# A relative-position bias made by four engines: double evacuations, a moved table load and other shares of the last tiles

## The reference

```python
batch, n_heads, seq, head_dim = 4, 8, 576, 64      # hidden = 32
scores = scale * np.matmul(q, k.transpose(0, 1, 3, 2))
rel = (pos[:, None] - pos[None, :]).astype(np.float32)
x = (np.log1p(np.abs(rel)) / psi_i)[..., None]
h = np.maximum(x @ w1 + b1, 0.0)                   # (seq, seq, 32)
bias = h @ w2                                      # (seq, seq, n_heads)
scores = scores + bias.transpose(2, 0, 1)[None]
attn = softmax(scores);  out = np.matmul(attn, v)
...
# then, on 2304 rows of 512: out += P[:, e:e+1] * (np.maximum(x @ w1[e], 0) @ w2[e]), e < 8
```

## Time and profile before

| what | value |
|---|---|
| median of 3 runs | 1846.01 us (1845.95 to 1847.39) |
| profiled execution | 1847.22 us, its span 1845.4 us |
| busy: PE, DVE, ACT, POOL | 99%, 57%, 45%, 56% of the span |
| granted TensorE clock, mean | 0.999 |
| bias part | from 5.4 us to the first scores at 61.3 us |

### The profile page before, as it was taken

How to read it: one execution, slowest core, us unless ns; L and a number is a source line. 1 busy time by engine, 2 the same in 40 slices (tenths; PEclk the granted TensorE clock), 3 DMA queues, 4 the chain that set the end, 5 groups by cost and what they waited for, 6 DMA issues and landing times.

```text
span 1845.4 us, 27892 instructions
## 1 busy us (share of the span) xinstructions
PE 1829.7 (99%) x10223; PEld 1592.1 (86%) x10223; DVE 1053.4 (57%) x1784; ACT 824.8 (45%) x1416; POOL 1028.3 (56%) x720
## 2 busy tenths in 40 slices
PE   8999999999999999999999999999999999999999
PEld 4677777788999999999999999999999999999998
DVE  8877777777554555456645554555455445544553
ACT  8777777533433333334333333333333333333331
POOL 0223326577666666666776666666666666666661
PEclk9999999999999999999999999999999999999999
DMA  7763562021112211212121211111121111112110
GB/s 241 226 155 92 128 152 68 23 79 59 69 69 69 69 69 69 69 69 103 69 69 69 69 69 69 69 69 69 69 103 69 69 69 69 69 69 69 69 46 35
DMA packets 44127, 152.47 MB, mean 83 GB/s; under 512 B 9584, under 2 KB 18032, under 8 KB 29680
## 3 DMA queue, kind: packets, MB, share of 16 engines
q1 hardware_dynamic: 44016, 150.99, 25.5%
HBM read 135.63 MB, written 15.34 MB: 82 GB/s over the span
## 4 chain that ended last, share of the span: by engine, by line
PE 94%; DVE 1%; ACT 1%; issue 0%; POOL 0%; ACTq 0%; DVEq 0%; POOLq 0%
PE banks L660 14%; PE banks L661 14%; PE banks L659 14%; PE banks L627 13%; PE banks L631 13%; PE banks L629 13%; PE banks L557 4%; PE banks L518 3%; PE banks L500 3%; PE banks L501 2%; PE banks L571 1%; PE banks L528 0%; DVE h_lo L1167 0%; PE banks L678 0%; ACT probs L786 0%
## 5 line engine op out<-in xcount | busy, mean ns | idle before, releaser
L1279 POOL TENSOR_TENSOR w_lo<-stage,w_hi 128x1024 fp32r<-128x1024 f32 (+1 forms) x288 | 647.5, 2263 | 526.8 <-ACT w_hi L832 525.9
L1161 DVE TENSOR_TENSOR u<-p_copy,banks 128x384 f32<-128x384 f32 x192 | 106.4, 554 | 633.3 <-PE banks L631 633.3
L661 PE MATMUL banks<-w_hi,h_lo 128*128 128x512 f32 x1152 | 450.1, 391 | 0.0
L660 PE MATMUL banks<-w_lo,h_hi 128*128 128x512 f32 x1152 | 449.9, 391 | 0.0
L659 PE MATMUL banks<-w_hi,h_hi 128*128 128x512 f32 x1152 | 449.0, 390 | 0.0
L1167 DVE SCALAR_TENSOR_TENSOR h_lo<-corner,h_hi 128x384 fp32r<-128x384 f32 x384 | 411.1, 1098 | 0.0
L879 ACT ACTIVATE h_hi<-corner 128x384 fp32r<-128x384 f32 x384 | 196.5, 526 | 271.1 <-DVE corner L1161 268.1
L627 PE MATMUL banks<-x_hi,w_hi 128*128 128x384 f32 x896 | 300.6, 336 | 0.6 <-DVE u L1161 0.6
L631 PE MATMUL banks<-x_hi,w_lo 128*128 128x384 f32 x896 | 300.2, 335 | 0.0
L832 ACT ACTIVATE w_hi<-stage 128x1024 fp32r<-128x1024 f32 (+1 forms) x288 | 271.6, 974 | 9.1 <-POOL stage L1273 9.1
L868 ACT ACTIVATE p_copy<-banks 128x384 f32<-128x384 f32 x96 | 47.3, 492 | 491.2 <-PE banks L631 491.2
(11 more groups left out here) (130 smaller groups left out, 2478.3 us busy)
## 6 DMA issues: line engine op xcount, KB each, us to landing
stage<-in_expert_w SPq DMA_DIRECT2D x96, 1024.0 KB, 4.7
raw<-in_qk SPq DMA_DIRECT2D x32, 576.0 KB, 7.1
bias_scratch<-bias_out SPq DMA_DIRECT2D x36, 288.0 KB, 2.6
bias<-bias_scratch SPq DMA_DIRECT2D x16, 288.0 KB, 2.9
v_main<-in_v SPq DMA_DIRECT2D x16, 256.0 KB, 2.7
bias<-bias_scratch SPq DMA_DIRECT2D x16, 256.0 KB, 4.0
out<-total SPq DMA_DIRECT2D x4, 768.0 KB, 4.0
out<-total SPq DMA_DIRECT2D x6, 256.0 KB, 2.0
```

The lines of the kernel that those rows point to most:

```text
L660: pe.matmul(dst, h_hi[:, g % 2, f, tokens], lo[:, f], start=False, stop=False)
L661: mm = pe.matmul(dst, h_lo[:, g % 2, f, tokens], hi[:, f], start=False, stop=fp == FPAIRS - 1 and f == 1)
L1161: dve.tensor_tensor(out, other, bank, op).then_inc(combined, 1)
L1279: pool.tensor_tensor(lo, of, hi.bitcast(F32), ALU.subtract).then_inc(w_split, 1)
```

## The change

ScalarE first does a dummy Relu on a column of `ones`, ahead of its waits, so that the activation table is loaded then. It runs two tiles ahead, and evacuates two tiles in one instruction of 128 x 1152 out of four banks, waiting for both tiles' matmuls and both slots' stores. In the last four tiles VectorE makes two units a tile and ScalarE two; these tiles have their own shift column `shift_last`. `bias_tile` on TensorE gets other waits for them, and the last round is written out after the loop. The low part of the first queries is made in two pieces: 128 columns of each head before the keys' low part, the rest after it, signalled by `first_split`, for which TensorE waits before step 1 and SyncE before `pairs_of`. Batch 1 is rounded by ScalarE, ahead of the exps of steps 0 and 1, in place of VectorE. VectorE no longer waits for `attn_consts_in` there.

```diff
+LAST_ROUND = BIAS_TILES - ROUND
+ON_VECTOR_LAST = GROUPS - 2
 # SyncE
+            sp.wait_ge(first_split, 1)
             with sp.Fori(0, PAIRS - 1) as hp:
                 pairs_of(hp, False)
 # TensorE
-            def bias_tile(m, slot):
+            def bias_tile(m, slot, last=False):
                 for first in range(0, GROUPS, 2):
-                    if first + 1 < ON_VECTOR:
+                    if last and first == 0:
+                        pe.wait_ge(hid_vec, ON_VECTOR * LAST_ROUND + ON_VECTOR_LAST * (slot + 1))
+                    elif last:
+                        pe.wait_ge(hid_act, LAST_ROUND + (GROUPS - ON_VECTOR_LAST) * (slot + 1))
+                    elif first + 1 < ON_VECTOR:
+            for slot in range(ROUND):
+                pe.wait_ge(bias_evac, LAST_ROUND - ROUND + slot + 1)
+                bias_tile(LAST_ROUND + slot, slot, last=True)
+                if not exists(hp, s - 2) and exists(hp, s - 1):
+                    pe.wait_ge(first_split, 1)
 # ScalarE
+            act.wait_ge(ones_set, 1)
+            act.activation(col_sum[:, 0:1], ones[:, 0:1], ACT.Relu).then_inc(warm, 1)
             act.wait_ge(consts_in, 48)
-            def keep_bias(m, slot, again=True):
-                act.wait_ge(bias_mm, GROUPS * (m + 1))
+            def keep_bias(m, slot, again=True, offset=shift):
+                act.wait_ge(bias_mm, GROUPS * (m + 2))
                 if again:
-                    act.wait_ge(bias_stored[slot], 16 // ROUND * (m - slot))
-                act.activation(halves(bias_out[:, slot, :]), banks[:, 2 * slot:2 * slot + 2, 0:HALF], ACT.Identity,
-                               bias=shift[:], scale=1.0 / SCALE).then_inc(bias_evac, 1)
+                    for of in range(2):
+                        act.wait_ge(bias_stored[slot + of], 16 // ROUND * (m - slot))
+                act.activation(bias_out[:, slot:slot + 2, :].rearrange("p t (a s) -> p (t a) s", a=2),
+                               banks[:, 2 * slot:2 * slot + 4, 0:HALF], ACT.Identity,
+                               bias=offset[:], scale=1.0 / SCALE).then_inc(bias_evac, 2)
-            for m in range(AHEAD):
+            for m in range(2):
                 hidden_units(m, m, again=False)
+            for m in range(LAST_ROUND - ROUND, BIAS_TILES, 2):
+                for of in range(2, 4):
+                    if m + of < BIAS_TILES:
+                        hidden_units(m + of, (m + of) % ROUND,
+                                     on_vector=ON_VECTOR_LAST if m + of >= LAST_ROUND else ON_VECTOR)
+                keep_bias(m, m % ROUND, offset=shift_last if m >= LAST_ROUND else shift)
             for s in range(STEPS):
+                if s < 2:
+                    round_pair(1, 1, s)
                 step(0, s)
 # VectorE
+            for slot in range(ROUND):
+                hidden_units(LAST_ROUND + slot, slot, again=True, on_vector=ON_VECTOR_LAST)
-            dve.wait_ge(attn_consts_in, 16)
             dve.wait_ge(rounded, 2)
+            split_first_queries(slice(0, P), split_done)
             dve.tensor_tensor(k_lo[0][:, :, :], raw[:, 0, 1, :, :], qk_hi[0][:, 1, :, :].bitcast(F32),
                               ALU.subtract).then_inc(split_done, 1)
+            split_first_queries(slice(P, S), first_split)
             for s in range(STEPS):
                 step(0, s)
-                if s < 2:
-                    dve.wait_ge(raw_in[1], 32)
-                    dve.tensor_copy(qk_hi[1][:, :, s, :], raw[:, 1, :, s, :]).then_inc(rounded, 1)
```

More of the change, by code:

```diff
@@ L473, in _ @@
                 bias_tile(m, m)
-            with pe.Fori(1, BIAS_TILES // ROUND) as i:
+            with pe.Fori(1, BIAS_TILES // ROUND - 1) as i:
                 for slot in range(ROUND):
@@ L736, in _, with hidden_units @@
         def _(act):
+            act.wait_ge(ones_set, 1)
+            act.activation(col_sum[:, 0:1], ones[:, 0:1], ACT.Relu).then_inc(warm, 1)
             act.wait_ge(consts_in, 48)
             act.wait_ge(bias_prep, 3)
-            def hidden_units(m, slot, again=True):
-                j = ON_VECTOR
+            def hidden_units(m, slot, again=True, on_vector=ON_VECTOR):
                 if again:
                     act.wait_ge(bias_mm, GROUPS * (m - ROUND + 1))
-                start = LTAB - S - GROUPS * GROUPS * m - GROUPS * j
-                act.activation(hidden[:, GROUPS * slot + j, :], table[:, bass.ds(start, S)], ACT.Relu,
-                               bias=b1_col, scale=slopes[:, bass.ds(GROUPS * m + j, 1)]).then_inc(hid_act, 1)
-            def keep_bias(m, slot, again=True):
-                act.wait_ge(bias_mm, GROUPS * (m + 1))
-                if again:
-                    act.wait_ge(bias_stored[slot], 16 // ROUND * (m - slot))
-                act.activation(halves(bias_out[:, slot, :]), banks[:, 2 * slot:2 * slot + 2, 0:HALF], ACT.Identity,
-                               bias=shift[:], scale=1.0 / SCALE).then_inc(bias_evac, 1)
+                for j in range(on_vector, GROUPS):
+                    start = LTAB - S - GROUPS * GROUPS * m - GROUPS * j
+                    act.activation(hidden[:, GROUPS * slot + j, :], table[:, bass.ds(start, S)], ACT.Relu,
+                                   bias=b1_col, scale=slopes[:, bass.ds(GROUPS * m + j, 1)]).then_inc(hid_act, 1)
+            def keep_bias(m, slot, again=True, offset=shift):
+                act.wait_ge(bias_mm, GROUPS * (m + 2))
+                if again:
+                    for of in range(2):
[3 more added lines that the diff above has]
+                               bias=offset[:], scale=1.0 / SCALE).then_inc(bias_evac, 2)
             def round_pair(n, slot, h):
@@ L760, in round_pair @@
                 act.activation(qk_hi[slot][:, :, h, :], raw[:, slot, :, h, :], ACT.Copy).then_inc(rounded, 1)
-            for m in range(AHEAD):
+            for m in range(2):
                 hidden_units(m, m, again=False)
-            act.wait_ge(shift_kept, 2)
-            for m in range(ROUND):
-                hidden_units(m + AHEAD, (m + AHEAD) % ROUND, again=m + AHEAD >= ROUND)
+            act.wait_ge(shift_kept, 4)
+            for m in range(0, ROUND, 2):
+                for of in range(2, 4):
+                    hidden_units(m + of, (m + of) % ROUND, again=m + of >= ROUND)
                 keep_bias(m, m, again=False)
@@ L769, in _ @@
                 round_pair(0, 0, h)
-            with act.Fori(1, BIAS_TILES // ROUND - 1) as i:
-                for slot in range(ROUND):
-                    hidden_units(ROUND * i + slot + AHEAD, (slot + AHEAD) % ROUND)
+            with act.Fori(1, BIAS_TILES // ROUND - 2) as i:
+                for slot in range(0, ROUND, 2):
+                    for of in range(2, 4):
+                        hidden_units(ROUND * i + slot + of, (slot + of) % ROUND)
                     keep_bias(ROUND * i + slot, slot)
[L774 to L777, removed]
+            for m in range(LAST_ROUND - ROUND, BIAS_TILES, 2):
+                for of in range(2, 4):
+                    if m + of < BIAS_TILES:
+                        hidden_units(m + of, (m + of) % ROUND,
+                                     on_vector=ON_VECTOR_LAST if m + of >= LAST_ROUND else ON_VECTOR)
+                keep_bias(m, m % ROUND, offset=shift_last if m >= LAST_ROUND else shift)
             def step(hp, s, last=False):
@@ L973, in _ @@
             dve.memset(shift[:], 0.0).then_inc(shift_kept, 1)
+            dve.memset(shift_last[:], 0.0).then_inc(shift_kept, 1)
             dve.memset(row_sum[:], 1.0).then_inc(bias_prep, 1)
@@ L979, in _, with hidden_units @@
             dve.wait_ge(shift_ready, 1)
[L980 to L985, removed]
+            dve.wait_ge(shift_kept, 2)
+            for to, units in ((shift, ON_VECTOR), (shift_last, ON_VECTOR_LAST)):
+                dve.tensor_scalar(to[0:C * units, :], banks[0:C * units, 7, SHIFT_AT:SHIFT_AT + 1],
+                                  1.0 / SCALE, None, ALU.mult).then_inc(shift_kept, 1)
+            def hidden_units(m, slot, again=False, on_vector=ON_VECTOR):
+                for j in range(on_vector):
                     if again:
@@ L994, in _, with split_first_queries @@
                 hidden_units(m, m)
[L995 removed]
+            with dve.Fori(1, BIAS_TILES // ROUND - 1) as i:
                 for slot in range(ROUND):
                     hidden_units(ROUND * i + slot, slot, again=True)
[L1000 removed]
+            for slot in range(ROUND):
+                hidden_units(LAST_ROUND + slot, slot, again=True, on_vector=ON_VECTOR_LAST)
             dve.wait_ge(rounded, 2)
[L1002 to L1003 removed]
+            def split_first_queries(cols, done):
+                low = slice(D, 2 * D)
+                dve.tensor_tensor(qk_hi[0][low, 0, :, cols], raw[low, 0, 0, :, cols],
+                                  qk_hi[0][low, 0, :, cols].bitcast(F32), ALU.subtract).then_inc(done, 1)
+            split_first_queries(slice(0, P), split_done)
```

(1 more changed line is left out.)

4 lines of the change are left out of this document (3 added, 1 removed).

## The result

The changed kernel takes 1848.97 us (median of 20 runs, 1847.23 to 1850.04) against 1846.03 (20 runs, 1845.84 to 1847.63): a ratio of 1.0013, 95% interval 1.0007 to 1.0019, that is 1.3 to 3.5 us slower. Forecast were 1844.7 us and a range up to 1847.2. The profiled execution took 1849.14 us, its span 1847.4.

The account below looks back on a forecast made before the run. TensorE bounds the kernel, gapless once attention runs, so only an earlier start helps: 0.6 us from the bias part plus 0.8 from the casts, 1847.22 - 1.4 = 1845.8 profiled, median stated 1844.7; range 1842.8 to 1847.2.

Parts of the forecast that it names:

- rival (d): Bias part, ScalarE: a double evacuation costs as two (1.38 us); first scores 64.4, time 1848.3; chance 0.07.
- rival (c): Hand-over: ScalarE is not the limit, VectorE's 58.3 counts; scores at 58.4, time 1842.3; chance 0.06.
- 19.4. From there a pair costs ScalarE 1.52 + 1.12: Bias part: tile 1's store lands at 19.4, then 2.64 us a pair puts pair 28,29 at 51.1.
- Rival (e): Bias part: tile 1's store lands after 19.4, delaying ScalarE equally; 1.4 us cancels the gain (1846.0); chance 0.05.
- VectorE has no cast before step 2's additions: Start of attention: with casts moved to ScalarE, step 2's transposes start at 70.0, 0.8 us of gain from the casts.
- from here on TensorE has no gap: Attention after step 2's transposes: TensorE stays busy, so the 1.4 us gained stay to the end.
- this delay, with 0.4 us: Start of attention: first rounding ends at 62.85, after the first maximum at 62.4; 0.4 of 0.6 us given back.
- the bias of chunk 3, which I had called hidden: Start of attention: SyncE's bias loads of chunks 3 and 4 start 1 us later; chunk 3 is wanted near 69.
- The 15 double evacuations of the sum: ScalarE's bias part: the skill's estimate of 1.15 us would put the end of the sum 0.3 us later.
- rival (b): Last tiles and first scores: TensorE's clock falls sooner, net cost 1.0 to 1.4 us, time 1845.7 to 1846.1; chance 0.16.

Follow-up runs that it names:

- Eight slots: Changed kernel with eight slots in bias_out in place of four, an evacuation waiting for the store eight tiles back; 1846.79 us.
- full-clock profile: Kernel before the change, unchanged, profiled again in an execution where TensorE's clock does not fall; 1846.06 us (one run).
- that of two tiles, with slots enough: Changed kernel with eight bias_out slots, batch 1's casts on VectorE, ScalarE's second unit in the last two tiles only; 1845.05 us.

## Why the prediction was wrong

**Right.** VectorE's 104 units end at 56.58 (56.6), the keys' low part at 58.42 (58.3), the early table load is worth nothing, a double evacuation takes 1.21 us and holds ScalarE for 1.11 (1.22 and 1.12), a pair 2.62 (2.64). From pair 28,29 to the first scores it is 9.6 us (51.1 to 60.7: 9.6). ScalarE, not VectorE, sets the hand-over, and VectorE idles. Step 2's transposes start 9.14 us after the first scores (forecast: 70.0 less 60.7, 9.3). GpSimd's low parts end at 73.56, and nothing waits for them. The rival (d) of a dear double evacuation is out, and rival (c) too.

**The step that failed first: "19.4. From there a pair costs ScalarE 1.52 + 1.12".** Here I took the first landing as fixed by the queue, and then treated stores as free. Landings cost 0.76 us more than that at 20.16, and 0.73 and 0.85 us at 36.76 and 48.22: 2.34 in sum, which is 53.47 less 51.1 to the last few hundredths, and all of the miss at the first scores (63.10 for 60.7). Eight slots remove just that and restore the forecast hand-over. Rival (e) had the right mechanism but put it only at the first store, at a chance of 0.05. Even there the rows gave more than 19.4: a store issued at 13.5 that takes 6.6 lands at 20.1. The arithmetic stood open: an evacuation of two tiles starts only when the later store has landed. Evacuation 16,17 could have started at 36.0, pair 12,13 was done at 31.9, and the second of its stores went out at 33.0 behind a bias load: 3.0 us for a landing that took 3.7 there. Before the change a tile waits for one store, that of the tile four back, and no evacuation waited for one after 19 us.

**The second step: "VectorE has no cast before step 2's additions", priced at -0.8.** The runs show +0.5 for the roundings alone (before + roundings on ScalarE) and +1.06 from the first scores to the marker in the changed kernel (17.07 for 16.01). Two things were wrong with it.

The baseline was delayed by the clock. The transposes of step 2 at 71.38 start 10.08 us after the first scores, in an execution at half clock from 63 to 66 us. At full clock they start 8.80 after them (70.16 less 61.36). The casts are in the way at either clock: in the full-clock profile VectorE works without a gap from 62.27 to the end of step 2's additions, both casts among them, and ScalarE waits 0.7 us for step 2's maximum. But the forecast of 9.3, which the changed kernel met, is then no gain of 0.8 but a loss of 0.3 to 0.5.

And "from here on TensorE has no gap" failed. A rounding now stands ahead of step 1's exps in ScalarE's queue; the exps, the copy of step 0 and the transposes of step 1 behind them come later (by 0.5 with the roundings alone), TensorE's wait there grows from 0.73 to 1.33, VectorE stands 1.31 us and makes its addition of step 3 later, and TensorE waits 0.69 before step 3's transposes (75.12), where it has no such wait in the full-clock profile of before. From step 2's transposes to the marker it is 7.93 us in place of 7.21.

**Part of this is the late first exp.** The first rounding stands behind the last double evacuation, and step 0's first exp starts 2.26 us after the first scores (65.36), against 1.72 with the roundings alone on the kernel before (63.06). The prediction had this delay, with 0.4 us, but followed it only as far as step 2's transposes. It goes on: in all five profiles with the roundings on ScalarE the marker comes 14.80 to 14.84 us after that exp, whatever the exp's own delay (1.72 to 2.26). So of the 1.06 us, counted this way, 0.54 are the loss that the roundings bring by themselves and 0.52 the first exp, later by that much behind the double evacuation. With the casts on VectorE in the changed kernel there is still a loss of 0.54, but by another wait, of 0.45, for the bias of chunk 3, which I had called hidden.

**Sums.** Some figures of the prediction do not come out of its rows. TensorE is done 1.29 after VectorE's last unit (58.43 to 59.72), not 1.2. The 15 double evacuations of the sum at 0.027 us more each put its end 0.4 later, not 0.3. The 0.8 us of rival (b) cannot be had from eight matmuls at 0.687 for 0.406, whose durations overlap. None of these moves the forecast by more than 0.1.

**Rival (b), the clock,** went the other way: the windows of the changed kernel's profile from 50 to 68 us all show 1.00, with the last tiles spread as forecast. The Trainium skill, "TensorE: Matmul & The Clock Gate", section "HAM oscillation", says that idle gaps between bursts bring the slow clock back; here the profiles where it fell are all of kernels with 1.58 us of idling before the first scores (and the clock fell in four of these six), while it stayed full in all profiles with at most 1.2. That agrees, but idling does not decide it alone: the kernel before + roundings on ScalarE idles 1.58 us too, and none of its 11 times lies in an upper group. Nor is it clear that the other kernels are free of it: the slowest run of the changed kernel (1850.04, not profiled) has a mean granted clock of 0.999, as the upper group of before has. What the fall costs is 1.2 us (1847.27 against 1846.06).

**The sum against the full-clock profile of before,** span 1844.2: first scores -0.67 as planned, landings +2.4, start of attention +1.06, and 0.4 in the remaining 1767 us, which varied by 0.7 between these kernels for reasons that no run separates: +3.2, and the spans differ by 3.2. The medians differ by 2.9.

## What to carry to other kernels

When two results are moved by one instruction, each of its waits becomes the later of two; work out the slack of every slot from the end of one use, through the store that is issued last, to the start of the next, at the places where other loads stand in the queue. A profile attributes a wait for several semaphores to one of them: where the named engine was long done, look at the landings, and where times come in two groups, find out which group the profile is of before a chain in it is used as a baseline. Work taken off one engine's chain lands in another's queue: follow what stands behind it there for two or three steps, and not only to the instruction that gains. Work taken off a loaded engine is worth only what the next limit leaves: the share of four tiles lost 1.4 us, that of two tiles, with slots enough, gained 0.5.

## What the runs showed of the hardware

The granted clock reads 1.00 throughout the bias part, but TensorE's first matmuls take 0.687 us each, for about 3 us in the changed kernel (to 9.6) and about 5 us in the kernel before (to 11.4), and 0.406 after that: the column of granted clock alone does not show that slow start. A fall to half clock (the 1.2 GHz level) in one short stretch after the hand-over, 63 to 66.5 us, splits a kernel's times into two groups 1.3 us apart. In the changed kernel a store of 288 KB lands 2.1 to 2.8 us after its issue, 3.6 to 4.6 behind a bias load of 576 KB and 5.8 to 6.9 behind the input loads. With the stores' landings on the path, times spread over 2.8 us; with eight slots, over 0.2.
